# Slot-major pair features, with c loads of 32 outermost source rows and a separate load for the squares

## The reference

```
logits = x @ phi                                  # 4608 x 32
...                                               # slots -> experts -> slot_out, 32 x 512
c = softmax(logits, over the 32 slots)            # 4608 x 32
x = c @ slot_out                                  # 4608 x 512
a = x @ w1 ; b = x @ w2                           # 4608 x 1024
h = a * b @ w3
out = h @ w_out                                   # 4608 x 512
```

## Time and profile before

| | us |
|---|---|
| median of three runs | 414.09 |
| lowest, highest | 411.47, 415.52 |
| the profiled execution's own time | 415.16 |
| its span, in which all the rows lie | 413.4 |
| PE busy (share of the span) | 378.1 (91%) |
| POOL busy | 168.7 (41%) |
| DVE busy | 170.9 (41%) |
| ACT busy | 125.4 (30%) |
| q1, share of 16 DMA engines' span | 67.2% |

### The profile page before, as it was taken

How to read it: one execution, slowest core, us unless ns; L and a number is a source line. 1 busy time by engine, 2 the same in 40 slices (tenths; PEclk the granted TensorE clock), 3 DMA queues, 4 the chain that set the end, 5 groups by cost and what they waited for, 6 DMA issues and landing times.

```text
span 413.4 us, 10207 instructions
## 1 busy us (share of the span) xinstructions
PE 378.1 (91%) x4215; PEld 273.2 (66%) x4215; DVE 170.9 (41%) x276; ACT 125.4 (30%) x246; POOL 168.7 (41%) x157
## 2 busy tenths in 40 slices
PE   1899989887989898999999999699799999989896
PEld 1778677766777677464545444478588888778775
DVE  1455465355535454350031001699733225432450
ACT  1022312221322133322343212322624434423342
POOL 1242322123232321754445420399744536754470
PEclk9999999999999999999999999789999999999999
DMA  8998999799989989778599990422214444434432
GB/s 264 341 319 275 369 363 363 233 364 355 351 266 380 394 310 356 296 281 331 208 400 421 419 380 5 86 71 96 96 45 150 176 175 176 160 116 175 177 120 101
DMA packets 38088, 102.93 MB, mean 249 GB/s; under 512 B 3552, under 2 KB 7968, under 8 KB 34208
## 3 DMA queue, kind: packets, MB, share of 16 engines
q1 hardware_dynamic: 38048, 102.34, 67.2%
HBM read 92.00 MB, written 10.32 MB: 248 GB/s over the span
## 4 chain that ended last, share of the span: by engine, by line
PE 69%; DMA 14%; SPq 5%; issue 4%; POOL 3%; DVE 3%; ACT 1%; ACTq 0%; DVEq 0%; POOLq 0%
PE psum L950 14%; PE psum L761 12%; PE psum L776 7%; PE psum L654 7%; DMA pkg_sb<-in_tiles 7%; DMA c_sb<-c_rows 7%; PE psum L620 6%; PE psum L681 5%; PE psum L918 4%; PE psum L640 3%; PE psum L667 3%; PE psum L716 3%; PE psum L692 2%; POOL feat L586 2%; SPq L502 2%
## 5 line engine op out<-in xcount | busy, mean ns | idle before, releaser
L586 POOL TENSOR_TENSOR feat<-c_sb 128x512 f32<-128x512 f32 x45 | 62.6, 1415 | 45.6 <-DMA c_sb<-c_rows 29.6
L542 POOL TENSOR_TENSOR pkg_sb<-pkg_sb,const_sb 128x512 f32<-128x512 f32 x36 | 37.6, 1044 | 105.7 <-DMA pkg_sb<-in_tiles 105.7
L1135 DVE TENSOR_TENSOR weights_t<-psum,const_sb 128x512 f32<-128x512 f32 x72 | 46.3, 685 | 41.1 <-PE psum L620 33.6
L950 PE MATMUL psum<-m_hi,feat_hi 128*128 128x512 f32 x144 | 56.5, 393 | 5.1 <-ACT out_sb L1117 3.5
L950 PE MATMUL psum<-m_hi,feat_lo 128*128 128x512 f32 x144 | 56.1, 390 | 0.0
L950 PE MATMUL psum<-m_lo,feat_hi 128*128 128x512 f32 x144 | 56.0, 389 | 0.0
L394 DVE TENSOR_TENSOR feat_lo<-feat,feat_hi 128x512 fp32r<-128x512 f32 x32 | 28.4, 887 | 60.3 <-ACT feat_hi L1085 58.4
L620 PE MATMUL psum<-pkg_sb 64*64 64x64 f32 (+1 forms) x1152 | 36.1, 259 | 17.2 <-DMA pkg_sb<-in_tiles 15.4
L620 PEld LDWEIGHTS psum<-pkg_sb 64*64 64x64 f32 x1152 | 29.4, 137 | 24.3 <-DMA pkg_sb<-in_tiles 17.2
L1085 ACT CAST feat_hi<-feat 128x512 fp32r<-128x512 f32 x45 | 27.7, 623 | 55.7 <-POOL feat L586 55.7
L654 PE MATMUL psum<-weights_t,pkg_sb 128*64 128x128 f32 x576 | 40.8, 283 | 1.8 <-issue 1.8
(11 more groups left out here) (126 smaller groups left out, 551.5 us busy)
## 6 DMA issues: line engine op xcount, KB each, us to landing
pkg_sb<-in_tiles SPq DMA_DIRECT2D x76, 256.0 KB, 5.5
pkg_sb<-in_tiles SPq DMA_DIRECT2D x32, 512.0 KB, 5.8
unit_a<-in_units SPq DMA_DIRECT2D x11, 1024.0 KB, 7.5
unit_x<-in_units SPq DMA_DIRECT2D x9, 1024.0 KB, 6.9
c_sb<-c_rows SPq DMA_DIRECT2D x36, 256.0 KB
out<-out_sb SPq DMA_DIRECT2D x36, 256.0 KB, 7.0
fold_raw<-in_fold SPq DMA_DIRECT2D x12, 512.0 KB, 7.4
unit_a<-in_units SPq DMA_DIRECT2D x12, 512.0 KB, 6.6
```

The source lines that it names most:

```text
L542: nc.gpsimd.tensor_tensor(v_nat(t).rearrange("p (h d) -> p h d", h=HEADS), v_nat(t).rearrange("p (h d) -> p h d", h=HEADS), decay.unsqueez ...
L586: nc.gpsimd.tensor_tensor(feat[:, k, :], c_sb[:, s, x, :], c_sb[:, s, y, :], ALU.mult).then_inc(feat_ready, 1)
L950: last = mm(psum[:, OUT + b, :], x, y, start=(at == 0 and m == 0), stop=(at == 4 and m == 2))
L1135: tt(weights_t[:, (2 * t + odd) % 4, :].rearrange("p (k b n) -> p k b n", k=2, b=2), psum[:, odd, :].rearrange("p (k b n) -> p k b n", k=2 ...
```

## The change

The partition order of the feature groups 0 to 3 is turned from 32 * i + s to 4 * s + i. Four things follow from it:

- `load_c` gives its source pattern as 32 rows of the slots outermost, then the 4 shifts, then 512 tokens (before: the 4 shifts outermost, then the 32 slots). The bytes are the same, 128 rows of 2 KB a load.
- The squares, group 4, keep the old order. They get a fifth version of c, with its own load (source pattern 4 copies of the 32 slots, outermost count 4 with step 0). `FEATURES[4]` is (4, 4) in place of (0, 0), `c_sb` has five versions, and POOL waits for 40 counts a place and chunk in place of 32.
- `pair_terms` makes the rows of M in the new order. For the three first terms (256, 128 and 128 of 544 columns) the innermost run of the patterns is 4 elements with step 0, 1 or 2 (`shifted4`) where it was 32 neighbours. The fourth term (32 columns) stays.
- The constant `C_HALF` halves rows with p % 4 == 3 in place of p >= 96.

```diff
-        c_sb = place("c_sb", [P, 2, 4, CHUNK * P], at=top[1])
+        c_sb = place("c_sb", [P, 2, 5, CHUNK * P], at=top[1])
...
+        def shifted4(base, at, step, *outer):
+
+            return bass.AP(base.tensor, base.offset + at,
+                           [list(base.ap[0])] + [list(n) for n in outer] + [[1, SLOTS], [step, 4]])
+
...
-                (dst[:, 0:2 * P].rearrange("p (k i s) -> p k i s", k=2, s=SLOTS),
-                 shifted(plain, 0, (0, 2), (0, 4)), shifted(y, 1, (1, 2), (2, 4))),
-                (by_slots(dst[:, 2 * P:3 * P]), shifted(plain, 0, (0, 4)), shifted(y, 13, (1, 4))),
-                (by_slots(dst[:, 3 * P:4 * P]), shifted(x, 1, (2, 4)), shifted(y, 13, (1, 4))),
+                (dst[:, 0:2 * P].rearrange("p (k s i) -> p k s i", k=2, s=SLOTS),
+                 shifted4(plain, 0, 0, (0, 2)), shifted4(y, 1, 2, (1, 2))),
+                (dst[:, 2 * P:3 * P].rearrange("p (s i) -> p s i", s=SLOTS),
+                 shifted4(plain, 0, 0), shifted4(y, 13, 1)),
+                (dst[:, 3 * P:4 * P].rearrange("p (s i) -> p s i", s=SLOTS),
+                 shifted4(x, 1, 2), shifted4(y, 13, 1)),
...
-        FEATURES = ((0, 1), (0, 2), (0, 3), (1, 3), (0, 0))
+        FEATURES = ((0, 1), (0, 2), (0, 3), (1, 3), (4, 4))
...
+                base = c_rows[:, bass.ds(n * (CHUNK * P), CHUNK * P)]
                 for a, (at, step) in enumerate(C_SHIFTS):
-                    base = c_rows[:, bass.ds(n * (CHUNK * P), CHUNK * P)]
                     src = bass.AP(base.tensor, base.offset + at * TOKENS,
-                                  [[step * TOKENS, 4], [TOKENS, SLOTS], [1, CHUNK * P]])
+                                  [[TOKENS, SLOTS], [step * TOKENS, 4], [1, CHUNK * P]])
                     sp.dma_start(c_sb[:, s, a, :], src).then_inc(c_loaded[s], 16)
+                src = bass.AP(base.tensor, base.offset, [[0, 4], [TOKENS, SLOTS], [1, CHUNK * P]])
+                sp.dma_start(c_sb[:, s, 4, :], src).then_inc(c_loaded[s], 16)
...
-                pool.wait_ge(c_loaded[s], (n + (2 - s)) * 32)
+                pool.wait_ge(c_loaded[s], (n + (2 - s)) * 40)
...
-    c[:, C_HALF] = np.where(np.arange(P) >= 3 * SLOTS, 0.5, 1.0)
+    c[:, C_HALF] = np.where(np.arange(P) % 4 == 3, 0.5, 1.0)
```

## The result

| | before | changed kernel |
|---|---|---|
| median of 20 runs, us | 415.01 | 412.83 |
| lowest, highest | 411.47, 418.89 | 407.31, 415.48 |
| profiled execution, us (its span) | 415.16 (413.4) | 409.50 (407.7) |

The ratio of the times is 0.9908, with a 95% interval of 0.9883 to 0.9932: 0.9% faster, 3.8 us of 415 (2.8 to 4.9). In the whole document ratios and intervals are made from the fast executions of a kernel alone (of the changed kernel 16 of 20, median 411.3 us), while a median beside them is one of all its executions. Forecast were -3.9 us and 410.2 us, with a chance of 0.42 of a gain over 1%.

A forecast was written before the change was run, and what follows sets the result against it. The prediction took late c loads, confined to four DMA engines, to cost 4.66 us in a final stage otherwise paced by PE. -4.66 + 0.77 (DVE) + 0 (POOL) = -3.9 us from 414.09 gave 410.2 us, range 408.2 to 413.0.

The forecast's parts named there:

- What bounds the kernel: Final stage: PE sets 11.79 us a chunk, but late c loads stretch later chunks and cost 4.66 us.
- Four engines: Final stage: c loads run on four of 16 DMA engines, from outermost count 4; 32 outermost rows allow all 16.
- The squares' load hidden at 192 KB and 7.7 us: Final stage: busiest engines move 192 KB a chunk in 7.7 us, under PE's 11.79; fifth issue on SP also hidden.
- pair_terms on DVE, +0.2 us for each f and +0.77 on the path: Pair stage: step-2 reads cost 0 to 0.40 us for each f, middle +0.2; six uncovered less 0.43 wait give +0.77.
- my formula: Pair stage: DVE's added time for each f, times 6, minus a 0.43 us wait, delays the path.
- The Trainium skill's rule on adjacent pairs: DVE pair products: full rate only for runs of two or more adjacent words; estimated +0.27 us each f, +1.2 on path.
- pair_terms on POOL, 0: Pair stage: POOL's three changed products, 1.96 us for each f, take no longer in runs of 4.
- rival 4: Pair products cost neither engine anything and POOL gains 0.19 us for each f by its broadcast: -5.0, 409.1 us; chance 0.18.
- The total: Whole kernel: -4.66 + 0.77 + 0 = -3.9 us, giving 410.2 us.
- Rivals 1 and 2: Pair products: DVE's double or worse, 411.4 us, chance 0.21; POOL's take twice as long, 421.7 us, chance 0.08.
- rival 3: Final stage: c loads stay on four engines, 384 KB each a chunk, 15.8 us; about +18 us, 432; chance 0.03.

The follow-up runs named there:

- pairs_only: The kernel before with only the changed kernel's `pair_terms`, c loads as before; 415.56 us, ratio 0.9950.
- shifts_outermost: The changed kernel with the four loads' sources nested as before (4 shifts outermost, then 32 slots), squares' load kept; 432.54 us, ratio 1.0406 to before.
- pair_step_4: The changed kernel with step 4 in place of 2 in the pair products' reads; a single run, 407.58 us.

## Why the prediction was right, and where not

*What bounds the kernel.* Right in place and size. The late loads cost 4.68 us (4.66 from the rows), and pairs_only, which keeps them, keeps 4.2 of that (110.61 against 106.38).

*Four engines.* Right. It was an inference from a share of 0.26; the outermost counts 2, 4 and 8 with shares of 0.13, 0.26 and 0.53 bear it out, and the chunk spacing of shifts_outermost follows to 0.1 us from the bytes of the busiest engine, scaled from 320 KB in 13.2 us.

*The squares' load hidden at 192 KB and 7.7 us.* Right: without it and with it spread the final stage is 106.4. Only its issue was priced too high: 0.58 us, not 1.4.

*pair_terms on DVE, +0.2 us for each f and +0.77 on the path.* This is the term that failed, twice. Its size was taken in the middle between 0 and 0.40 and is 0: 415 ns against 414 for the 256 columns, 412 against 419 for the 128 that are read from `ab_ext` alone. Its way to the end was wrong too: pair_step_4 adds (0.575 - 0.415) + (0.494 - 0.412) = 0.24 us for each f, for which my formula gives 6 x 0.24 - 0.43 = +1.0, and 0.3 was measured. The formula let every delay of VectorE reach the final stage through PE's last block. But there PE waits 1.63 us in the changed kernel, and as long in the kernel before (1.61 from 297.54 in its chain), so that way was covered. The way that counts is the last sum, ACT and then GpSimd's four `feat_lo`, and on it the delay was 0.3.

The Trainium skill's rule on adjacent pairs ("Vector Engine (DVE) Microarchitecture Reference", measured stream behaviour) would have made it +1.2, by an estimate. At step 2 the trace does not bear the rule out (no cost). At step 4 it does, with 0.63 ns a column; the page's 1.75 against 1.054, measured with both sources hopping, makes 0.70. The measurement decides.

*pair_terms on POOL, 0.* Right, 739 ns against 771 and 620 against 615. The profiles with the new patterns at step 2 all have 736 to 742 ns where the one of before has 771, so 0.03 us for each f may be a gain; rival 4's 0.19 is not there.

*The total.* The sum -3.9 met the timed -3.8 by luck. By the stages the change is worth 4.68 us in the final stage and 0.1 ahead of it (1.1 to 1.2%), which the interval of 2.8 to 4.9 holds: the wrong +0.77 and a timed gain 1.0 short of the stages' happened to agree. The time itself, 412.83, is 2.6 above the forecast 410.2 and near the upper end of the range of 408.2 to 413.0; 0.9 of it is the kernel before, whose median went from 414.09 in three runs to 415.01 in twenty. Rival 4 (nothing on VectorE or GpSimd costs anything) is the case that came true, without the 0.38 of gain that it added. Rivals 1 and 2 fell with the pair stage's 131.45, where before had 131.55, and rival 3 with the share. shifts_outermost built rival 3 on purpose: its +18 us above the kernel before was measured as +17 (432.54 against 415.78).

## What to carry to other kernels

A DMA share that sat flat at a round part of 16 engines (0.13, 0.26, 0.53) was here each time the sign of loads confined by their pattern. Divide the bytes of each DMA by the number of engines that its pattern allows, sum for the busiest engine over one period, turn that into time by a measured rate of the same kind of load, and compare with the pace of the engine that consumes: that gives both whether a nesting matters and how much, and it tells which loads may stay confined. Where the stages ahead scatter by several us from run to run, read an edit from the length of the stages it touches, and use the ratios for effects that are large beside their scatter.

## What I had not expected of the hardware

- VectorE and GpSimd read one source at a step of 2 words (8 bytes) no slower than neighbours, in runs of only 4 elements (415 and 739 ns for 256 columns); a step of 4 words costs 160 and 101 ns more.
- The attention stage's end moved by 7.4 us (164.5 to 171.9) between profiles, and by 4.6 us (166.7 and 171.3) between two of one program. What makes it scatter was not tried.
- Long PE waits cost a second time: with loads on two engines PE stood idle for 12.63 us ahead of the last chunk, the granted clock was 0.55 from 500 to 510 us, and the last chunk took 14.27 us instead of 12.08.
